# Attention and two feed-forward layers in one kernel: column halves from even and odd tiles, value sums on 32 array columns, denominators by tensor_reduce

## The chip, the cores and the metric

One Trainium2 chip, one NeuronCore of it. The metric is the device time of one execution of the whole program in microseconds (us). The kernel before takes 609.03 us, the median of 3 runs (608.67 to 610.44).

## The reference

Everything is float32. Three stages follow one another; `B, H, S, D = 2, 8, 768, 64`, so there are 1536 tokens of 512 values.

```python
k_sum = k.reshape(B, H, nb, 32, D).max(axis=3)          # nb = 24 blocks of 32 keys
v_sum = v.reshape(B, H, nb, 32, D).mean(axis=3)
scores = concat(where(abs(i - j) < 16, scale * q @ k.T, -1e9), scale * q @ k_sum.T + log(32))
a = exp(scores - max); a = a / (sum(a) + 1e-9)
x = a @ concat(v, v_sum)                                # attention, [1536, 512]
y = silu(x @ w_gate) * (x @ w_val) @ w_out              # hidden width 1536
h = y @ w_in                                            # hidden width 2048
out = where(h >= 1, h, where(h <= -1, 0, (h + 1)**2 / 4)) @ w_out2
```

## The kernel before

**Attention.** A group is one batch, 768 tokens, in 12 tiles of 64 queries (`QT`). A tile sees 96 keys and 24 block sums, padded to 128 columns. For tile `s` (0 to 11 in group 0) the engines do in turn: `first_scores` on TensorE (L536), `mask_scores` on VectorE (L1117), four `exponentials` on ScalarE with their totals (L843), `inverses` on VectorE (L1125, which adds 1e-9 to the totals by a tensor_scalar, and L1127), `normalise` on GpSimd (L1394), `transposes` on TensorE (L557), `copy_trans` on ScalarE (L856) and `values` on TensorE (L579). `values` wants in rows 96 to 127 of its operand `v_s` (group 0) or `v_a` (group 1) the 24 block means of v. `value_sums` (L517) makes these: six matmuls of 128 by 512 per group, with a selection matrix `sel` as weights, into rows 96 to 127 of one PSUM bank. For group 0 they stand in the PE's order at tiles 3, 4 and 5 (`SUMS_WITH`), and VectorE copies them out (`place_v_sum`, L1105 and L1106); three DMAs of the SP queue (L387) spread them to the other tiles. For group 1 they stand between the first products of the feed-forward stage, and ScalarE copies them (L826) and issues two DMAs for them (L831).

**Feed-forward.** Each group's x, 512 by 768, is cut into 2 by 2 blocks, rows by rows and columns by columns (`T` is 384 tokens), and multiplied by a 7-product scheme with sums and differences of blocks. `raw` holds x. `x_sum` (L1155, VectorE) makes the differences T1 to T4, `x_part_hi` (L884, ScalarE) rounds each of seven blocks to float32r in `x_hi`, and `x_part_lo` (L1163, VectorE) leaves the remainder in `x_lo`; each product is six matmuls (L589). The products of a unit `u` are p1, p2, p4 of the unit before, p6, p3 of the unit before, p5 and p7, in the order of the loop. The first one of a phase waits for the block of x that it reads (`x_needed`). In group 0 the columns 0 to 383 are tiles 0 to 5, so that B11 and B21 (all that p1 and p2 read) are ready after tile 5.

There are four phases `k`: group 0 and group 1 through the gated layer, then both through the second. While phase 0 runs, the attention of group 1 (tiles 12 to 23) runs between its products. Each phase ends in the second matmul of its layer (L698 for k below 2, L726 after), and `evacuate` copies the accumulators out of PSUM. In phases 2 and 3 these are six tiles of 128 tokens by 512, in `y_out`.

**The SP queue.** All loads and stores but the two of L831 are issued by SP, in one written order. `load_w(u)` (L429) brings the weights of a unit in two transfers, into one of three buffers; `load_wout` (L437) the second matmul's; `store(k)` (L444) issues six stores of 128 rows of 2 KB from `y_out` as the accumulators come out. `store(2)` stands in SP's order before the loads of units 3 to 7 of phase 3, `store(3)` at the end.

```python
def store(k):
    g = k % 2
    for j in range(len(ACC2)):
        sp.wait_ge(*evacuated(k, j))
        row = g * S + j * P
        sp.dma_start(out[row:row + P, :], y_out[g][:, j]).then_inc(stored, 16)
```

**ScalarE and VectorE in a unit.** ScalarE does for unit `u` in turn: `u3_copy(u-1)`, `p1_copy(u)`, `w_hi_a(u+1)` (which waits for `load_w(u+1)`), `take_c21(u-1)`, `u2_copy(u)`. p7(u) waits for `u2_copy(u)`.

Of the kernel before, what the change touches and what calls it, by code (L numbers as in the profile page):

```python
# [9 lines left out]
ACT = mybir.ActivationFunctionType  # L10
# [3 lines left out]
P = 128  # L14
# [21 lines left out]
SEL0 = WIN + (VCH - 1) * (P // BLOCK)  # L36
# [13 lines left out]

T = S // 2
T_A = T - 2 * QT
# [18 lines left out]
SLOTS_T = 9  # L71
# [38 lines left out]
def build(nc, q_t, k_t, v_rows, w1, w2, out):  # L110
    ctx = ExitStack()
    with ctx:
# [22 lines left out]
        prob_tx = at("prob_tx", 18432, [SLOTS_T - 5, PAIRS, P])  # L135
# [3 lines left out]
        k_raw_b = [at(f"k_raw_b{c}", o, [S // SUB // 3 * PAIRS * SUB]) for c, o in enumerate((152576, 156672, 189440))]  # L139
# [14 lines left out]
        v_sum = at("v_sum", 193536, [B, DM])  # L154
        masked = at("masked", 197632, [2, PAIRS, COLS])
        sel = at("sel", 201728, [SEL0 - WIN + P])
# [6 lines left out]
        total = at("total", 212544, [RING, PAIRS])  # L163
        denom = at("denom", 212608, [RING, PAIRS])
        inv = at("inv", 212672, [RING, PAIRS])
        half = at("half", 212736, [1])
# [86 lines left out]
        v_pair_sums = sem("v_pair_sums")  # L253
        v_first_sums = [sem(f"v_first_sums{j}") for j in range(len(SUMS_AT))]
        v_late_loaded = [sem(f"v_late_loaded{j}") for j in range(2)]
        v_late_sums = [sem(f"v_late_sums{j}") for j in range(2)]
# [87 lines left out]
        def x_count(k, m, part=1):  # L344
            if k == 0:
                return {X_B11: 1, X_B21: 2, X_T2: 3 + part, X_T1: 5 + part}.get(m, m + 3)
            return 7 * k + m + 3

        def t_count(k, i, part=1):
            return 4 * k + i + 3 if k or i >= 2 else i + 1 + 2 * part  # L350

        def part_cols(k, m, part):
            return slice(0, T) if k or m not in (X_T1, X_T2) else (slice(0, T_A), slice(T_A, T))[part]

# [7 lines left out]
        def _(sp):  # L362
# [10 lines left out]
            def load_v_tok(b):  # L373
                src = v_rows[b, WINDOW:WINDOW + S, :].rearrange("(c p) d -> p c d", p=P)
                for c in range(0, VCH, 2):
                    sp.dma_start((v_tok_a, v_tok_b)[b][:, c:c + 2], src[:, c:c + 2]).then_inc(v_tok_loaded[b][c // 2], 16)
# [5 lines left out]

            def place_first_sums(j):
                if j == 0:
                    sp.wait_ge(v_sum_ready, 1)
                c0, c1 = SUMS_AT[j]
                sp.dma_start(v_s[WIN:, c0:c1], v_sum[WIN:, 0].unsqueeze(1).to_broadcast([P - WIN, c1 - c0, DM])  # L387
                             ).then_inc(v_first_sums[j], 16)
# [63 lines left out]
            load_q(2)  # L452
            load_q(3)
            load_v(0)
            load_q(4)
            load_v(1)
            load_q(5)
            load_v(2)
            load_w(1)
            load_v(3)  # L460
            place_first_sums(0)
            place_first_sums(1)
            place_first_sums(2)
# [14 lines left out]
            load_late(7)  # L478
            load_w(4)
# [28 lines left out]
        def _(pe):  # L508
            def value_sums(b, i):
# [9 lines left out]
                if i == VCH - 1:  # L519
# [40 lines left out]
            def values(s, dst):  # L560
                v, c0 = v_slots(s // 2)
                r = c0 + s % 2
                if s % 2 == 0:
                    pr = s // 2
                    pe.wait_ge(v_first_loaded[pr] if pr < FIRST else v_late_loaded[pr % 2], v_count(pr))
                    if s == 0:
                        pe.wait_ge(v_pair_sums, 1)
                    for j, (c0, _) in enumerate(SUMS_AT):
                        if s == c0:
# [923 lines left out]
```

## Time and profile before

| | us |
|---|---|
| median of 3 runs | 609.03 |
| lowest and highest run | 608.67, 610.44 |
| the profiled execution, its own time | 608.4 |
| its span | 606.3 |
| TensorE matmul busy | 586.3 |
| VectorE busy | 469.5 |
| ScalarE busy | 363.2 |
| GpSimd busy | 86.4 |

The span runs from the first to the last recorded event; 2.1 us of the execution's own time lie around it. The granted TensorE clock has a mean of 0.997. Busy times are shares of the span by engine; weight loads of TensorE (PEld) overlap its matmuls.

### The profile page before, as it was taken

To read this page: it belongs to the slowest core of one execution; us is meant where nothing else is said; L and a number is where in the kernel's file an instruction comes from. 1 tells how busy PE (TensorE), PEld (TensorE's weight loads), DVE (VectorE), ACT (ScalarE), POOL (GpSimd) and SP (SyncE) were. 2 spreads that over 40 slices of the span, in tenths; PEclk is the share of its full clock that TensorE was granted. 3 is DMA by queue.
4 is the path that set the end of the run, shared out by engine and by line. 5 is a ranking of instruction groups with operands and counts; after the bars stand their busy time and mean duration, and the time that the engine had idled before them with its cause. 6 is when DMAs were issued, how large, how long until landed. Compare 5 with 4: busy or idle time off the path is not lost.

```text
span 606.3 us, 10568 instructions
## 1 busy us (share of the span) xinstructions
PE 586.3 (97%) x3912; PEld 540.4 (89%) x3912; DVE 469.5 (77%) x906; ACT 363.2 (60%) x733; POOL 86.4 (14%) x80
## 2 busy tenths in 40 slices
PE   3989999999999999999999999999999999999997
PEld 3667789989899999999999999998878899998886
DVE  6789788988585667778776767998998479979833
ACT  4776888888755456666634545664655456655522
POOL 3760232432300002232210000000000000000000
PEclk9989999999999999999999999999999999999999
DMA  9985442442122112223212111321111323002212
GB/s 331 242 302 159 129 138 79 132 131 97 53 61 62 53 35 70 71 69 122 88 53 70 53 36 69 122 88 46 60 52 53 139 70 122 2 35 73 67 53 104
DMA packets 31330, 57.50 MB, mean 95 GB/s; under 512 B 3184, under 2 KB 5744, under 8 KB 31280
## 3 DMA queue, kind: packets, MB, share of 16 engines
q1 hardware_dynamic: 31120, 56.57, 28.8%
q8 instruction: 31, 0.51, 0.4%
q10 hardware_dynamic: 160, 0.26, 0.2%
q14 instruction: 19, 0.16, 0.1%
HBM read 52.23 MB, written 3.15 MB: 91 GB/s over the span
## 4 chain that ended last, share of the span: by engine, by line
PE 82%; DVE 9%; ACT 5%; issue 2%; DMA 1%; POOL 0%; ACTq 0%; POOLq 0%; SPq 0%; DVEq 0%
PE ps L589 45%; PE ps L726 18%; PE ps L698 15%; ACT prob_s L843 1%; DVE hid_lo L1231 1%; PE ps L557 1%; PE ps L579 1%; DMA k_raw<-k_t_dram 1%; PE ps L550 1%; DVE rel L1237 1%; PE ps L517 1%; DVE h L1240 1%; DVE x_lo L1163 1%; DVE wout_lo L1225 1%; ACT prob L843 1%
## 5 line engine op out<-in xcount | busy, mean ns | idle before, releaser
L589 PE MATMUL ps<-x_hi,w_hi 128*128 128x384 f32 x560 | 192.1, 343 | 1.3 <-DVE h L1219 0.4
L589 PE MATMUL ps<-x_lo,w_hi 128*128 128x384 f32 x560 | 187.4, 335 | 0.0
L589 PE MATMUL ps<-x_hi,w_lo 128*128 128x384 f32 x560 | 187.2, 334 | 0.0
L589 PEld LDWEIGHTS ps<-x_hi,w_hi 128*128 128x128 f32 x560 | 105.1, 188 | 6.0 <-issue 3.7
L589 PEld LDWEIGHTS ps<-x_hi,w_lo 128*128 128x128 f32 x560 | 105.2, 188 | 1.1 <-issue 1.0
L589 PEld LDWEIGHTS ps<-x_lo,w_hi 128*128 128x128 f32 x560 | 105.1, 188 | 0.0
L962 ACT ACTIVATE wout_hi<-wout_raw 128x512 fp32r<-128x512 f32 x56 | 35.3, 631 | 95.1 <-PE ps L726 52.0
L726 PE MATMUL ps<-wout_hi,hid_hi 128*128 128x512 f32 x192 | 74.8, 390 | 0.8 <-DVE wout_lo L1225 0.8
L726 PE MATMUL ps<-wout_hi,hid_lo 128*128 128x512 f32 x192 | 75.2, 392 | 0.1
L726 PE MATMUL ps<-wout_lo,hid_hi 128*128 128x512 f32 x192 | 74.8, 389 | 0.0
L1225 DVE TENSOR_TENSOR wout_lo<-wout_raw,wout_hi 128x512 fp32r<-128x512 f32 x56 | 39.4, 704 | 40.1 <-ACT wout_hi L962 39.6
L1404 POOL TENSOR_TENSOR h<-part,silu 128x384 f32<-128x384 f32 x36 | 47.8, 1333 | 135.7 <-ACT silu L954 90.2
L698 PE MATMUL ps<-hid_lo,wout_hi 128*128 128x384 f32 x192 | 64.5, 336 | 0.6 <-DVE hid_lo L1231 0.6
L698 PE MATMUL ps<-hid_hi,wout_hi 128*128 128x384 f32 x192 | 64.3, 335 | 0.7 <-DVE wout_lo L1225 0.7
L698 PE MATMUL ps<-hid_hi,wout_lo 128*128 128x384 f32 x192 | 64.2, 334 | 0.0
L1188 DVE TENSOR_TENSOR w_lo<-w_sum,w_hi 128x1024 fp32r<-128x1024 f32 x39 | 47.5, 1219 | 14.7 <-ACT w_hi L898 14.7
L1231 DVE TENSOR_TENSOR hid_lo<-h,hid_hi 128x768 fp32r<-128x768 f32 x56 | 53.5, 956 | 1.5
L975 ACT ACTIVATE hid_hi<-h 128x768 fp32r<-128x768 f32 x56 | 46.6, 833 | 2.4 <-DVE h L1240 2.4
L898 ACT ACTIVATE w_hi<-w_sum 128x1024 fp32r<-128x1024 f32 x40 | 42.2, 1055 | 7.4 <-PE ps L589 5.1
L726 PEld LDWEIGHTS ps<-wout_hi,hid_lo 128*128 128x128 f32 x192 | 36.0, 188 | 8.6 <-DVE hid_lo L1231 1.2
L726 PEld LDWEIGHTS ps<-wout_hi,hid_hi 128*128 128x128 f32 x192 | 36.0, 188 | 8.3 <-issue 1.1
L726 PEld LDWEIGHTS ps<-wout_lo,hid_hi 128*128 128x128 f32 x192 | 36.0, 188 | 7.5
(119 smaller groups left out, 925.6 us busy)
## 6 DMA issues: line engine op xcount, KB each, us to landing
w_raw<-w_dram SPq DMA_DIRECT2D x80, 256.0 KB, 2.9
wout_raw<-w_dram SPq DMA_DIRECT2D x56, 256.0 KB, 2.6
out_dram<-y_out SPq DMA_DIRECT2D x12, 256.0 KB, 2.1
v_s<-v_rows_dram SPq DMA_DIRECT2D x6, 384.0 KB, 11.9
v_a<-v_rows_dram SPq DMA_DIRECT2D x6, 384.0 KB, 3.7
v_tok_a<-v_rows_dram SPq DMA_DIRECT2D x3, 512.0 KB, 7.9
k_raw_b<-k_t_dram SPq DMA_DIRECT2D x3, 512.0 KB, 7.5
v_tok_b<-v_rows_dram SPq DMA_DIRECT2D x3, 512.0 KB, 9.4
```

Of the source, the lines that this page charges most:

```text
L517: last = nc.tensor.matmul(v_sum_ps[b][:], sel[:, c0:c0 + P], (v_tok_a, v_tok_b)[b][:, i], start=i == 0, stop=i == VCH - 1)
L589: last = nc.tensor.matmul(dst, lhs, rhs, start=start and kk == 0 and i == 0, stop=kk == 1 and i == 2, skip_group_check=not start)
L698: last = nc.tensor.matmul(bank[ACC1[j]][:, 0:T], lhs, rhs, start=i == 0 and e == 0, stop=ends and e == 2)
L726: last = nc.tensor.matmul(bank[ACC2[j]][:], lhs, rhs, start=i == 0 and e == 0, stop=ends and e == 2)
L843: last = nc.scalar.activation(prob_of(s)[:, a], masked[:, s % 2, a], ACT.Exp, scale=-1.0, bias=neg_max[:, c, a:a + 1], accum_out=total[:, ...
L898: nc.scalar.activation(w_hi[:, u % 2, W_S2:W_S4 + 1], w_sum[:], ACT.Copy).then_inc(ws_hi, 1)
L962: nc.scalar.activation(wout_hi[:, n % 2], wout_raw[:, n % RAWS], ACT.Copy).then_inc(wout_hi_ready, 1)
L975: nc.scalar.activation(hid_hi[:, n % 2], h[:, c], ACT.Copy).then_inc(hid_hi_ready, 1)
L1188: nc.vector.tensor_tensor(w_lo[:, u % 2, W_S2:W_S4 + 1], w_sum[:], w_hi[:, u % 2, W_S2:W_S4 + 1], ALU.subtract).then_inc(ws_lo, 1)
L1225: nc.vector.tensor_tensor(wout_lo[:, n % 2], wout_raw[:, n % RAWS], wout_hi[:, n % 2], ALU.subtract).then_inc(wout_lo_ready, 1)
L1231: nc.vector.tensor_tensor(hid_lo[:, n % 2], h[:, c], hid_hi[:, n % 2], ALU.subtract).then_inc(hid_lo_ready, 1)
L1404: nc.gpsimd.tensor_tensor(dst, part[:, u % 2, c], silu[:, c], ALU.mult).then_inc(h_pool, 1)
```

## The change

1. **Order of tokens.** In a group's `raw`, columns 0 to 383 now hold the even tiles and 384 to 767 the odd ones. So `first_copy_out` and `late_copy_out` write other columns, and every block of x needs tiles from all over the group. The result comes out in that order, and `store` puts each 128 rows back in two runs of 64 rows, 128 rows apart.
2. **Token operands of phase 0** are made in two column ranges (`PARTS`, the tiles of pairs 0 to 3 and of pairs 4 and 5), each for groups of blocks at once: B11 with B21, then all four differences, then B22.
3. **Value sums** are made on 32 array columns: three steps of four matmuls of 32 by 256, each in another 32 rows of PSUM, at tiles 2 and 3 for group 0. One copy of 128 by 256 takes them out into `v_part`, and four DMAs of 12 or 20 partitions put them where they belong. For group 1 these are SP's too, behind `load_late(7)`.
4. **Denominators**: the totals stand beside a constant 1e-9, and a tensor_reduce adds the two in place of the tensor_scalar.
5. GpSimd's weight sums of unit 0 come ahead of tile 0, SP loads `v_s` in another order, and some buffers lie elsewhere (`prob_tx`, `k_raw_b`).

```diff
-T_A = T - 2 * QT
+PARTS = (slice(0, 4 * QT), slice(4 * QT, T))
+PART_PAIRS = (4, 6)
+X_GROUPS = ((0, 2), (2, 6), (6, 7))
+HI_ORDER = ((0, 0), (0, 1), (1, 0), (1, 1), (0, 2), (1, 2))
+LO_ORDER = ((0, 0), (1, 0), (0, 1), (1, 1), (0, 2), (1, 2))
-SUMS_WITH = {3: (0, 1), 4: (2, 3), 5: (4, 5)}
-SUMS_AT = ((2, 4), (4, 8), (8, TILES))
+SUMS_WITH = {2: (0, 1), 3: (2,)}
+SUMS_AT = ((0, 6), (6, TILES))
...
+            def place_sums(b, dst, ready):
+                for j in range(4):
+                    half, y = divmod(j, 2)
+                    n = P - WIN - VHALF if half else VHALF
+                    row = WIN + half * VHALF
+                    part_of = v_part[BLOCK * j:BLOCK * j + n, b].unsqueeze(1).to_broadcast([n, dst.shape[1], DM // 2])
+                    sp.dma_start(dst[row:row + n, :, y * (DM // 2):(y + 1) * (DM // 2)], part_of).then_inc(ready, 16)
...
             def store(k):
                 g = k % 2
                 for j in range(len(ACC2)):
                     sp.wait_ge(*evacuated(k, j))
-                    row = g * S + j * P
-                    sp.dma_start(out[row:row + P, :], y_out[g][:, j]).then_inc(stored, 16)
+                    half, c = divmod(j, T // P)
+                    rows = out[g * S + (4 * c + half) * QT:g * S + (4 * c + half + 1) * QT, :]
+                    both = bass.AP(rows.tensor, rows.offset, [(2 * QT * DM, 2), (DM, QT), (1, DM)])
+                    sp.dma_start(both, y_out[g][:, j]).then_inc(stored, 16)
...
-                if i % 2 == 0:
-                    pe.wait_ge(v_tok_loaded[b][i // 2], 16)
-                c0 = SEL0 - WIN - i * (P // BLOCK)
-                last = nc.tensor.matmul(v_sum_ps[b][:], sel[:, c0:c0 + P], (v_tok_a, v_tok_b)[b][:, i],
-                                        start=i == 0, stop=i == VCH - 1)
+                pe.wait_ge(v_tok_loaded[b][i], 16)
+                c0 = SEL0 - i * (P // BLOCK)
+                for j in range(4):
+                    half, y = divmod(j, 2)
+                    last = nc.tensor.matmul(v_sum_ps[b][BLOCK * j:BLOCK * j + BLOCK, 0:DM // 2], sel[:, c0:c0 + BLOCK],
+                                            (v_tok_a, v_tok_b)[b][:, half * (VCH // 2) + i, y * (DM // 2):(y + 1) * (DM // 2)],
+                                            start=i == 0, stop=i == VCH // 2 - 1)
...
-                c = (s - LAST_A) * QT
+                c = s % 2 * T + (s - LAST_A) // 2 * QT
                 nc.scalar.activation(raw[1][:, :, c:c + QT], tile_out(AT1), ACT.Copy).then_inc(late_out, 1)
...
-                nc.vector.tensor_scalar(denom[:, c], total[:, c], 1e-9, None, ALU.add).then_inc(denom_ready, 1)
+                nc.vector.tensor_reduce(denom[:, c], total[:, c], AX.X, ALU.add).then_inc(denom_ready, 1)
...
+            def x_first_lo(part, group):
+                dve.wait_ge(x_hi_ready, HI_ORDER.index((part, group)) + 1)
+                if group:
+                    dve.wait_ge(scores_done, LAST_A)
+                lo, hi = X_GROUPS[group]
+                nc.vector.tensor_tensor(x_lo[:, lo:hi, :, PARTS[part]], x_first(raw[0], part, group),
+                                        x_hi[:, lo:hi, :, PARTS[part]], ALU.subtract).then_inc(x_lo_ready, 1)
```

**Three places in the order.** First SP, from the second matmul's loads of phase 2 to the end. Before:

```order
L437 DMA wout_raw<-w_dram 128x512 x13
L444 DMA out_dram<-y_out_55 128x512 x6
L429 DMA w_raw<-w_dram 128x512 x10
L437 DMA wout_raw<-w_dram 128x512 x16
L444 DMA out_dram<-y_out_56 128x512 x6
```

And changed:

```order
L465 DMA wout_raw<-w_dram 128x512 x13
L474 DMA out_dram<-y_out_55 2x64x512 x6
L457 DMA w_raw<-w_dram 128x512 x10
L465 DMA wout_raw<-w_dram 128x512 x16
L474 DMA out_dram<-y_out_56 2x64x512 x6
```

Nothing has moved; the destination of each store has three dimensions, 2 by 64 by 512, where it had 128 by 512. Its source is still 128 partitions by 512.

Second, VectorE where group 0's attention ends and its x operands are made (`k_sum` rows are the key maxima of group 1). Before:

```order
L1101 TENSOR_REDUCE k_sum<-k_raw_b_70 128x4x8
L1125 TENSOR_SCALAR denom<-total 128x4
L1127 RECIPROCAL inv<-denom 128x4
...
L1163 TENSOR_TENSOR x_lo<-raw_53,x_hi 128x768
...
L1163 TENSOR_TENSOR x_lo<-raw_53,x_hi 128x768
L1101 TENSOR_REDUCE k_sum<-k_raw_b_71 128x4x8
L1155 TENSOR_TENSOR t_first<-raw_53 128x2x256
```

And changed:

```order
L1165 TENSOR_TENSOR t_first<-raw_53 128x2x256
L1165 TENSOR_TENSOR t_first<-raw_53,t_first 128x2x256
L1173 TENSOR_TENSOR x_lo<-raw_53,x_hi 128x4x256
L1121 TENSOR_REDUCE k_sum<-k_raw_b_71 128x4x8
...
L1165 TENSOR_TENSOR t_first<-raw_53 128x2x128
L1165 TENSOR_TENSOR t_first<-raw_53,t_first 128x2x128
L1173 TENSOR_TENSOR x_lo<-raw_53,x_hi 128x4x128
...
L1173 TENSOR_TENSOR x_lo<-t_first,x_hi 128x8x256
```

The remainder that the first product needs stood right behind the copy of pair 3; it is now complete only with the range of 128 columns, behind the four differences of the first range, a key maximum and the copy of pair 5.

Third, TensorE at tiles 3 and 4 of group 0 (`q_b` are queries, `ident` rows transposes). Before:

```order
L536 MATMUL ps<-k_raw,q_a 64x96 x4
L536 MATMUL ps<-k_sum,q_a 64x32 x4
L557 MATMUL ps<-ident,prob_s 128x128 x4
L517 MATMUL ps<-v_tok_a,sel 128x512 x2
L536 MATMUL ps<-k_raw,q_b 64x96 x4
```

And changed:

```order
L569 MATMUL ps<-k_raw,q_a 64x96 x4
L569 MATMUL ps<-k_sum,q_a 64x32 x4
L549 MATMUL ps<-v_tok_a,sel 32x256 x4
L590 MATMUL ps<-ident,prob_s 128x128 x4
L569 MATMUL ps<-k_raw,q_b 64x96 x4
```

The value sums stand ahead of the first transposes instead of behind three of them.

## Rows read from the trace of the kernel before

**Rows 1.** Busy time by stretch (us): engine busy, PEclk, DMA share, GB/s.

```profile
18.00:21.00 3.00, 3.00 (x41) 1.72 (x41) 1.47 (x11) 2.13 (x9) 2.47 (x4) 1.00 1.06 308
...
24.00:27.00 3.00, 3.00 (x93) 2.61 (x96) 2.65 (x19) 2.01 (x8) 1.12 (x3) 1.00 0.68 141
27.00:30.00 3.00, 3.00 (x94) 2.62 (x88) 2.67 (x14) 3.00 (x12) 1.95 (x3) 1.00 0.98 253
...
40.00:41.00 1.00, 1.00 (x17) 0.88 (x14) 1.00 (x2) 1.00 (x2) 0.57 (x1) 0.50 1.05 385
...
43.00:44.00 1.00, 1.00 (x16) 0.69 (x13) 1.00 (x2) 0.00 (x0) 0.00 (x0) 1.00 0.14 51
```

**Rows 2.** Timeline of PE, 0 to 75 us: start, duration, what.

```profile
14.82 1.88 PE L517 MATMUL ps<-v_tok_a,sel 128*128 128x512 f32 x4
...
24.69 0.69 PE L579 MATMUL ps<-prob_ts,v_s 128*64 128x64 f32 x16
...
43.33 1.98 PE L517 MATMUL ps<-v_tok_b,sel 128*128 128x512 f32 x4
...
48.56 0.74 PE L589 MATMUL ps<-x_hi,w_hi 128*128 128x384 f32 x1
...
56.01 0.67 PE L550 MATMUL ps<-k_a,q_a 64*64 64x128 f32 x16
...
62.77 0.63 PE L557 MATMUL ps<-ident,prob 128*128 128x128 f32 x4 [0.99 <-POOL prob L1394]
```

**Rows 3.** Timeline of ACT: the copy behind the last exponentials of group 0.

```profile
38.37 0.58 ACT L856 ACTIVATE prob_ts<-ps 128x512 f32<-128x512 f32 x1
```

**Rows 4.** Timeline of DVE: a denominator that waits, and work behind it.

```profile
32.25 0.88 DVE L1125 TENSOR_SCALAR denom<-total 128x4 f32<-128x4 f32 x1 [1.17 <-ACT prob_s L843]
...
41.91 0.94 DVE L1163 TENSOR_TENSOR x_lo<-raw,x_hi 128x768 fp32r<-128x768 f32 x1
...
46.62 0.42 DVE L1155 TENSOR_TENSOR t_first<-raw 128x256 f32<-128x256 f32 x1
...
49.39 1.21 DVE L1101 TENSOR_REDUCE k_sum<-k_raw_b 128x32 f32<-128x1024 f32 x1
...
55.30 0.95 DVE L1163 TENSOR_TENSOR x_lo<-raw,x_hi 128x768 fp32r<-128x768 f32 x1
```

**Rows 5.** Timeline of POOL at the same time.

```profile
30.75 2.37 POOL L1436 TENSOR_TENSOR w_lo<-w_sum,w_hi 128x1024 fp32r<-128x1024 f32 x1
```

**Rows 6.** DMA issues, 0 to 110 us: KB each, median us to landing.

```profile
k_a<-k_sum SPq DMA_DIRECT2D x2, 128.0 KB, 4.6
```

**Rows 7.** Timeline of SP: the stores and the weights behind them.

```profile
476.72 3.83 SPq L444 DMA_DIRECT2D out_dram<-y_out  x6
480.59 28.61 SPq L429 DMA_DIRECT2D w_raw<-w_dram  x10
```

**Rows 8.** The last six stores: timeline of SP.

```profile
600.37 3.83 SPq L444 DMA_DIRECT2D out_dram<-y_out  x6
```

**Rows 9.** DMA, 600.7 to 605.8 us: 40 slices, packets, queue and issues.

```profile
DMA  0000899995789999999999998999899999999300
...
DMA packets 864, 1.57 MB, mean 308 GB/s; under 512 B 96, under 2 KB 96, under 8 KB 864
...
q1 hardware_dynamic: 864, 1.57, 82.5%
...
out_dram<-y_out SPq DMA_DIRECT2D x6, 256.0 KB, 2.1
```

**Rows 10.** The whole span: the queue of ScalarE's two DMAs.

```profile
q10 hardware_dynamic: 160, 0.26, 0.2%
```

**Rows 11.** Timeline of ACT in unit 2 of phase 3.

```profile
493.43 0.63 ACT L891 ACTIVATE w_hi<-w_raw 128x512 fp32r<-128x512 f32 x1
```

**Rows 12.** Timeline of PE in the same unit: the first matmul of p7.

```profile
498.04 0.33 PE L589 MATMUL ps<-x_hi,w_hi 128*128 128x384 f32 x1
```

More of the change, by code:

```diff
@@ L162, in build @@
         neg_max = at("neg_max", 212480, [RING, PAIRS])
[L163 to L166, printed above, removed]
+        total = at("total", 212544, [RING, PAIRS, 2])
+        denom = at("denom", 212672, [RING, PAIRS])
+        inv = at("inv", 212736, [RING, PAIRS])
+        half = at("half", 212800, [1])
         ps = ctx.enter_context(nc.psum_tensor("ps", [P, 8, 512], F32))
@@ L341, in evacuated, with x_count, t_at, x_first @@
             return (evac_act, evac_dve)[j % 2], (0, 4, 8, 11)[k] + j // 2 + 1
-        def x_count(k, m, part=1):
+        def x_count(k, m):
             if k == 0:
-                return {X_B11: 1, X_B21: 2, X_T2: 3 + part, X_T1: 5 + part}.get(m, m + 3)
-            return 7 * k + m + 3
+                group = [lo <= m < hi for lo, hi in X_GROUPS].index(True)
+                return 1 + max(LO_ORDER.index((part, group)) for part in range(2))
+            return 7 * k + m
         def t_count(k, i, part=1):
-            return 4 * k + i + 3 if k or i >= 2 else i + 1 + 2 * part
-        def part_cols(k, m, part):
-            return slice(0, T) if k or m not in (X_T1, X_T2) else (slice(0, T_A), slice(T_A, T))[part]
+            return 4 * k + i + 5 if k else 4 * part + i + 1
+        def t_at(i):
+            return (1, 0, 2, 3)[i]
+        def x_first(raw0, part, group):
+            cols = PARTS[part]
+            if group == 0:
+                return raw0[:, :, cols].rearrange("p (m k) c -> p m k c", m=2)
+            if group == 1:
+                return t_first[:, :, :, cols]
+            return raw0[:, 2:4, T + cols.start:T + cols.stop].unsqueeze(1)
         def block_of(k, i):
@@ L748, in _ @@
                 first_scores(s)
+                for i in SUMS_WITH.get(s, ()):
+                    value_sums(0, i)
                 now = VALUES_AT.get(s, ())
@@ L755, in _ @@
                     first_values(i)
-                for i in SUMS_WITH.get(s, ()):
-                    value_sums(0, i)
             first_transposes(LAST_A - 3)
@@ L859, in late_copy_out, with x_first_hi, x_part_hi @@
                 act.wait_ge(attn_done, s + 1)
-                c = (s - LAST_A) * QT
+                c = s % 2 * T + (s - LAST_A) // 2 * QT
                 nc.scalar.activation(raw[1][:, :, c:c + QT], tile_out(AT1), ACT.Copy).then_inc(late_out, 1)
-            def x_part_hi(k, m, part=1):
+            def x_first_hi(part, group):
+                act.wait_ge(first_out, PART_PAIRS[part])
+                if group == 1:
+                    act.wait_ge(t_ready, t_count(0, 3, part))
+                lo, hi = X_GROUPS[group]
+                nc.scalar.activation(x_hi[:, lo:hi, :, PARTS[part]], x_first(raw[0], part, group), ACT.Copy).then_inc(x_hi_ready, 1)
+            def x_part_hi(k, m):
                 r = raw[k % 2]
                 if m in (X_B11, X_B21, X_B22):
-                    if k == 0:
-                        act.wait_ge(first_out, FIRST if m == X_B22 else FIRST // 2)
-                    elif k == 1:
+                    if k == 1:
                         act.wait_ge(late_out, LAST_A)
@@ L1439, in _ @@
             pool.wait_ge(selected, steps)
+            for step in range(3):
+                first_weight_sums(0, step)
             for s in range(LAST_A):
                 normalise(s)
-                if 1 <= s <= 3:
-                    first_weight_sums(0, s - 1)
-                elif s == 4:
+                if s == 1:
                     first_w_lo_a()
-                elif s == 5:
+                elif s == 3:
                     first_w_lo_b()
```

202 lines of the change are left out of this document (96 added, 106 removed).

## The prediction

> **What bounds the kernel now.** I read the busy time by stretch first, then the timelines of PE, ACT and DVE up to 75 us, then the SP queue and its DMAs at the two places where results are stored. Three stretches differ.
>
> *Attention of group 0, up to 39 us.* ScalarE should set the pace, and from 27 us on it does: 3.00 busy of 3.00. Before that PE holds it up: in the three stretches of 3 us from 18 to 27 (the first and the last are shown) ScalarE is busy 2.13, 2.13 and 2.01 [rows 1]. What PE does there is value sums, 1.88 us for two matmuls of 128 by 512 [rows 2].
>
> *The passage to the feed-forward stage, 39 to 76 us.* VectorE works without a gap on x operands; the matmuls follow it. PE runs on a granted clock of 0.50 for some 3 us here, which is its level of 1.2 GHz, after two thin microseconds, and is back at 1.00 by 43 us [rows 1].
>
> *From 76 us to the end* PE is the bound, and little waits. So this part has a fixed length, unless a change starves it. The stores hide under it in phase 2; in phase 3 they are the tail: SP issues the last six from 600.37 us on [rows 8], and the data move from 601.2 to 605.4 (the slices from the fifth to the 38th) [rows 9].
>
> **The change part by part.**
>
> *Value sums.* Two of the old matmuls cost 1.88 us [rows 2], so one of the new, with half the columns, 0.47 us, and a group has twelve. If the four of a step run side by side, a group costs 3 x 0.47 = 1.4 us in place of 5.6; if not, the same 5.6. That matmuls on different array columns do overlap shows in the value matmuls: 8 with 64 columns would be 8 x 64/512 x 0.94 = 0.94 us one behind the other, and take 0.69 [rows 2]. I take 1.4.
>
> *Attention of group 0.* ScalarE's waits of 18 to 27 us go (0.87 + 0.87 + 0.99 = 2.7 us). So do the long denominators: the one at 32.25 lasts 0.88 us and ends at 33.13, when the GpSimd instruction of 30.75 ends (33.12) [rows 4, 5]. A tensor_reduce of 128 by 8 has no row here; between nothing gained and all of that wait, 0 to 0.7 us for each such case, I take 0.5 once. ScalarE then is done with the exponentials of tile 11 at about 35 instead of 38.4 [rows 3].
>
> *The passage.* Here 3.4 us are mostly given back. p1 of unit 0 needed the first half of the tokens, and now needs all. Behind the copy of pair 3, at 35.4, VectorE has to do: three copies (0.6 each), four differences of 512 columns (0.6), the remainder of 1024 (1.1), a key maximum (1.1), two differences of 256 (0.35) and a remainder of 512 (0.6), 7.7 us, and 0.5 of waiting for GpSimd. The prices go by columns: 768 cost 0.95, 256 cost 0.42, a key maximum 1.21 [rows 4], less some 0.08 by which neighbours overlap. p1 starts at 43.8. p6 needs another 4.7 us of VectorE's work and starts at 48.5, where it started at 48.56 before [rows 2]. So nearly nothing is won up to there. The two value sums behind it shrink by 0.4 us each. The scores of tile 12 (56.01 before [rows 2]) now wait for the last key maximum, done at about 51.0, and its transfer, 4.6 us [rows 6]: 55.6, a gain of 0.4. VectorE has then finished the x operands (before at 56.2, the end of the remainder at 55.30 [rows 4]), so tile 12's softmax runs without delay, and its transpose moves from 62.77 [rows 2] to 60.5. Its values wait for four small DMAs of SP. I keep **2.0 us** of gain. Ends: VectorE's finish moves by 5.2 us (56.2 to 51.0), a gain of at most 5; and a loss of 1.5, if PE, idle from 39.3 to 43.8, starts the stage at 1.2 GHz and the loss does not fit into its 2 us of slack ahead of p6.
>
> *The stores.* This is the term that decides. Today six stores are 864 packets, 144 each: 128 rows and 16 more. ScalarE's two transfers are 160, 80 each: 64 rows and 16 more [rows 9, 10]. So each is cut into sixteen, over all 16 DMA engines. In each transfer of before that I looked at the outermost count is the same on both sides (128, 96 or 32 partitions). The new store has 128 outermost at its source and 2 at its destination. No row shows such a transfer. Bounds: sixteen engines as today, or two. I take **two**, as that is the only outermost count by which both sides can be cut. The six stores take 0.825 x 16 x 5.1 us = 67.3 engine-us for 1.57 MB [rows 9], so one engine moves 23.4 GB/s, and two move the six stores in 67.3 / 2 = **33.7 us**, in place of 4.2.
>
> The Trainium skill, page "DMA: Bandwidth & Descriptors", section "Why a DMA increments its semaphore by 16 and not by 1", says that a transfer is split by the largest number up to 16 that divides the slowest dimension of both sides, so two here. With the page's 27 GiB/s of an engine the stores would take 27 us, by my estimate, and the total would be 642 us. The packets of both transfers agree with the split; none shows a small one.
>
> *At the end*: the data end at 601.2 + 33.7 = 634.9 instead of 605.4: **+29.5 us**.
>
> *In the middle*: `store(2)` is issued from 476.72, the data start 0.85 us later (as at the end), at 477.6, and end at 511.3. Behind it SP issues the weights of unit 3 of phase 3, from 480.59 [rows 7]. They use all engines, the two busy ones among them, and queue there behind the stores; then 2 x 16 KB for each engine at 23.4 GB/s, 1.4 us, and 0.6 to land: 513.3. ScalarE wants them at 493.43 [rows 11] and stands; behind `w_hi_a` stand `take_c21` and `u2_copy` (1.4 us for the three), and p7 of unit 2 waits for the last. PE gets there at 498.04 [rows 12] and goes on at 514.7: 16.7 us. Its clock will be at 1.2 GHz then, as it was around 40 us; there it lasted some 3.4 us (it is at 1.00 again in the stretch from 43 [rows 1]), half of which is lost: 1.7. Together **+18.4 us**.
>
> *Sum*: 608.4 - 2.0 + 29.5 + 18.4 = 654.3 for the profiled execution. The median stands 0.6 above it: **655**.
>
> *Costed at nothing*: the sums of unit 0 on GpSimd (it has nothing else to do before the first denominators), the column order in the late copies (the same elements), SP's new order of loads (the value sums that it waits for are ready sooner, so the loads behind them are issued sooner too). If that cover goes, each is worth under 1 us.
>
> **The rivals.**
>
> 1. *Only the end pays.* Later loads pass the stores on the two engines, or come in time. Against it: one queue carries both. Time: 609.0 - 2.0 + 29.5 = 636.5.
> 2. *The stores still go to 16 engines*, the 128 partitions of the source setting the split. This ends on the other side, and the point is the number n of engines: the end costs 67.3/n - 4.2, the middle nothing from n = 4 on. From 11 engines up the end costs under 2 us and the gain of 2.0 wins. With 16: 607.0.
> 3. *Sixteen engines, and the clock takes the gain.* With value sums gone PE is busy for some 1.2 us of each 2.0 in tiles 4 to 7, and idle for 4.5 us ahead of p1. The granted clock fell after a stretch like that once [rows 1]. Then transposes and scores take twice as long, about ScalarE's own pace, and p1 and p2 2 us more: 610.5.
>
> The Trainium skill, page "TensorE: Matmul & The Clock Gate", Part 1, has the clock fall to half after a spell without work, which would favour 3 over 2; the row at 40 us agrees with it, and it leaves my sum as it is, where the loss stands already.
>
> **How the numbers follow.** Forecast 0.80; rival 1 0.07; rival 2 0.09; rival 3 0.04. A measurement of this kernel tells 0.3% (1.8 us) from nothing: faster 0.08 (most of rival 2), same 0.03, slower 0.89. The range of the forecast itself goes by the speed of one engine. Both places take the six stores' time: at 27 us for them (one engine a quarter faster) the total is 642, and at 39 us (a seventh slower) 666; 2 us more for the front's ends. With rival 1 it reaches down to 636. Left out are rivals 2 and 3, 0.13, and the tails. Range **636 to 668**.
>
> **What would show it.** Two engines: the landing time of `out_dram` rises from 2.1 us to over 20 for the last; the six stores have 130 packets each; the DMA share after 605 us is near 2/16; a wait of PE of some 16 us on the weights of unit 3 of phase 3, with a granted clock of 0.5 behind it. The front: value sums of about 0.5 us a step; p1 of unit 0 near 43.8, and PE's steady stretch starting 2 us earlier. I would be wrong if stores keep 144 packets; partly, if the weights of unit 3 land on time.

## Result and the profile after

| | before | changed |
|---|---|---|
| median | 609.54 us (4 runs, 608.67 to 610.44) | 659.05 us (4 runs, 657.2 to 663.36) |
| profiled execution: own time, span | 608.4, 606.3 us | 660.64, 658.9 us |
| granted clock, mean | 0.997 | 0.953 |

Ratio **1.0814** (95% interval 1.0787 to 1.084): 49.5 us slower. The forecast was 655.0 (636 to 668), slower.

Three marks divide both spans: the first issue of `store(2)`, that of `store(3)`, and the end. The timeline of SP of the changed kernel has them; [rows 7, 8] are the same rows of before.

```profile
16.50 3.49 SPq L405 DMA_DIRECT2D v_s<-v_part  x4
...
21.82 3.27 SPq L405 DMA_DIRECT2D v_s<-v_part  x4
...
484.21 20.12 SPq L474 DMA_DIRECT2D out_dram<-y_out  x6
504.37 29.38 SPq L457 DMA_DIRECT2D w_raw<-w_dram  x10
...
624.93 19.96 SPq L474 DMA_DIRECT2D out_dram<-y_out  x6
```

| part | before | changed | difference | predicted |
|---|---|---|---|---|
| front, to `store(2)` | 476.72 | 484.21 | +7.5 | -2.0 |
| middle, to `store(3)` | 123.65 | 140.72 | +17.1 | +18.4 |
| end | 5.93 | 33.97 | +28.0 | +29.5 |

The end, in the DMA view of 624 to 658.9 us: 40 slices of busy tenths, then their rates, packets, queue and issues. It answers to [rows 9].

```profile
DMA  0010111111111111111111111111111111111110
GB/s 0 0 19 28 28 38 52 52 52 49 49 52 52 61 52 52 52 52 52 47 52 52 52 52 52 52 52 52 49 49 52 52 52 52 52 52 52 52 49 2
DMA packets 781, 1.58 MB, mean 45 GB/s; under 512 B 12, under 2 KB 12, under 8 KB 780
...
q1 hardware_dynamic: 780, 1.57, 12.0%
```

The data move from the third slice to the 39th, 625.7 to 658.0: 32.3 us, where 4.2 were. The same 1.57 MB now go at 52 GB/s in the full slices; over its whole window, idle slices included, this view has a mean of 45 where [rows 9] have 308. The small packets are 12 for six stores, two a store, where [rows 9] have 96, sixteen a store. The engines were busy for 0.120 x 16 x 34.9 = 67.0 engine-us, as before (67.3): the work is the same, done by two instead of sixteen.

The middle, in the timelines of ACT and PE. They answer to [rows 11, 12].

```profile
519.18 0.63 ACT L917 ACTIVATE w_hi<-w_raw 128x512 fp32r<-128x512 f32 x1 [18.16 <-DMA w_raw<-w_dram]
```

```profile
520.62 0.69 PE L620 MATMUL ps<-x_hi,w_hi 128*128 128x384 f32 x1 [14.93 <-ACT part L954]
521.11 0.52 PE L620 MATMUL ps<-x_hi,w_lo 128*128 128x384 f32 x1
```

ScalarE waits 18.2 us for the weights behind the stores, PE 14.9 us for ScalarE, and its matmuls then take 0.52 us instead of 0.33: the granted clock is 0.50 from 520 to 524 us, and 1.00 again from 526 on. Against the first issue of `store(2)`, p7 starts 15.1 us later than before (36.4 us behind it, not 21.3); the other 2.0 us of the middle come with this clock.

The front, by stretch (busy time of PE, PEld, DVE, ACT, POOL, then granted clock, DMA share, GB/s). It answers to [rows 1].

```profile
21.00:24.00 3.00, 2.47 (x68) 2.16 (x68) 1.18 (x10) 1.92 (x9) 0.69 (x2) 0.83 1.06 153
24.00:27.00 3.00, 1.67 (x19) 1.58 (x20) 1.27 (x10) 1.02 (x6) 1.71 (x2) 0.50 1.01 218
27.00:30.00 3.00, 3.00 (x59) 2.49 (x59) 0.85 (x2) 2.46 (x10) 0.00 (x0) 0.54 1.07 162
```

And what PE did there, and at p1 of unit 0 (the first row answers to the first of [rows 2]):

```profile
12.27 1.26 PE L549 MATMUL ps<-v_tok_a,sel 128*32 128x256 f32 x16
14.15 0.64 PE L549 MATMUL ps<-v_tok_a,sel 128*32 128x256 f32 x8
...
21.51 0.40 PE L569 MATMUL ps<-k_raw,q_b 64*64 64x96 f32 x8 [2.01 <-DMA q_b<-q_t_dram]
25.34 1.12 PE L610 MATMUL ps<-prob_ts,v_s 128*64 128x64 f32 x16 [1.36 <-issue]
...
34.05 0.38 PE L569 MATMUL ps<-k_raw,q_d 64*64 64x96 f32 x3
36.62 0.43 PE L569 MATMUL ps<-k_raw,q_d 64*64 64x96 f32 x3 [2.20 <-issue]
...
52.74 0.66 PE L620 MATMUL ps<-x_hi,w_hi 128*128 128x384 f32 x1 [4.57 <-issue]
53.19 0.52 PE L620 MATMUL ps<-x_hi,w_lo 128*128 128x384 f32 x1
```

DVE at tile 11's denominator, first before and then changed, with the copy of pair 3 behind it:

```profile
38.50 0.74 DVE L1125 TENSOR_SCALAR denom<-total 128x4 f32<-128x4 f32 x1 [0.31 <-ACT prob_s L843]
...
43.56 0.16 DVE L1143 TENSOR_REDUCE denom<-total 128x4 f32<-128x8 f32 x1 [0.93 <-ACT prob_s L865]
...
43.85 0.66 DVE L1150 COPY raw<-ps 128x512 f32<-128x512 f32 x1
```

The value sums did become cheap, 1.9 us in place of 5.6. But ScalarE, which should have gained by it, is busy 1.92 and 1.02 of 3.00; PE waits for transfers, its clock goes to 0.50, and the DMA engines are busy all the time while they move 153 to 218 GB/s, where the first of [rows 1] has 308 at the same share. The denominator of tile 11 comes at 43.56 us, not at 38.50, and tile 12's transposes at 70.11, not at 62.77. So 5.1 us of the front are lost in group 0's attention and 2.3 in the passage.

The wait before 25.34 ends when the value sums are there. The DMA view in steps of 1 us counts rows of 1 KB, which in this stretch are those of the sums alone: of the 384 rows for tiles 0 to 5, issued from 16.50 on, the first moves after 18 us, 383 have moved by 24 and the last by 25.

The wait of 2.20 us at 36.62 is of another kind: it stands inside the scores of one tile, where the program has no wait. It comes up again below.

### The profile page after: what moved, and what is told of

It reads as the page before. It is cut to its first block, busy times and chain, and to the rows that moved or that the text cites. A ratio compares the mean times of both kernels' runs of the same rounds, so it can differ in the third digit from the quotient of the medians.

```text
span 658.9 us, 10625 instructions
## 1 busy us (share of the span) xinstructions
PE 587.1 (89%) x3936; PEld 543.1 (82%) x3936; DVE 465.8 (71%) x905; ACT 363.0 (55%) x730; POOL 86.6 (13%) x80
## 4 chain that ended last, share of the span: by engine, by line
PE 78%; DVE 5%; SPq 4%; DMA 4%; issue 3%; ACT 1%; POOL 0%; POOLq 0%; ACTq 0%; DVEq 0%
PE ps L620 42%; PE ps L757 16%; PE ps L729 14%; SPq L474 3%; DMA q_b<-q_t_dram 2%; PE ps L610 2%; PE ps L590 2%; DMA w_raw<-w_dram 1%; DVE hid_lo L1264 1%; PE ps L583 1%; PE ps L569 1%; SPq L457 1%; DVE rel L1270 1%; DVE h L1273 1%; DVE t_late L1190 1%
## 5 line engine op out<-in xcount | busy, mean ns | idle before, releaser
L620 PE MATMUL ps<-x_hi,w_hi 128*128 128x384 f32 x560 | 192.6, 344 | 19.9 <-ACT part L954 14.9
L988 ACT ACTIVATE wout_hi<-wout_raw 128x512 fp32r<-128x512 f32 x56 | 35.3, 631 | 95.1 <-PE ps L757 52.0
```

Source lines behind the costliest of these rows:

```text
L620: last = nc.tensor.matmul(dst, lhs, rhs, start=start and kk == 0 and i == 0, stop=kk == 1 and i == 2, skip_group_check=not start)
L988: nc.scalar.activation(wout_hi[:, n % 2], wout_raw[:, n % RAWS], ACT.Copy).then_inc(wout_hi_ready, 1)
```

## The experiments

Of the forecast, the two store terms had to be shown and the front explained. Times are medians; "front" is the first issue of `store(2)` in the profiled execution, against 476.72. The front of one and the same program moves by up to 2.5 us from one execution to another (the changed kernel, split stores and split middle are the same there: 484.21, 484.92 and 486.67), so medians weigh more than a single front.

### Split stores

```diff
-                    both = bass.AP(rows.tensor, rows.offset, [(2 * QT * DM, 2), (DM, QT), (1, DM)])
-                    sp.dma_start(both, y_out[g][:, j]).then_inc(stored, 16)
+                    for i in range(2):
+                        r0 = g * S + (4 * c + half + 2 * i) * QT
+                        sp.dma_start(out[r0:r0 + QT, :], y_out[g][i * QT:(i + 1) * QT, j]).then_inc(stored, 16)
```

> The changed kernel with each of its twelve stores made as two transfers of 64 partitions, each to one run of 64 rows of the output, instead of one transfer of 128 partitions whose destination has three dimensions. Output is the same. Theory (the three-dimensional destination spreads a store over two DMA engines only): the end falls back from 34.0 us behind the first issue of the second group of stores to about 6, the stretch between the two groups of stores from 140.7 to about 123.6, and what is left is the later start of the first group (+7.5): 659.0 - 28.0 - 17.1 = 614 us (611 to 618). Rival (the stores are slow for another reason, the 512-column rows or the W loads beside them): the time stays within 3 us of 659.

Measured: **619.91 us** (617.46 to 621.88; before beside it 608.91; ratio 1.0166, 1.0128 to 1.0205).

```profile
484.92 7.62 SPq L474 DMA_DIRECT2D out_dram<-y_out  x12
...
608.58 7.52 SPq L474 DMA_DIRECT2D out_dram<-y_out  x12
```

The middle is 608.58 - 484.92 = 123.66, as before: the whole term is gone. The end is 618.2 - 608.58 = 9.6, so 24.4 of 28.0 are gone; 3.7 stay, since the twelve issues in a row take 7.52 us where the six of before took 3.83. That, and a front 0.7 us later, are 4.4 of the 6 us between 620 and the expected 614; the other 1.6 are that 614 was reckoned from the median, 659.05, with terms from an execution of 660.64.

### The new destination alone, in the kernel before

```diff
-                    row = g * S + j * P
-                    sp.dma_start(out[row:row + P, :], y_out[g][:, j]).then_inc(stored, 16)
+                    half, c = divmod(j, T // P)
+                    rows = out[g * S + (4 * c + half) * QT:g * S + (4 * c + half + 1) * QT, :]
+                    both = bass.AP(rows.tensor, rows.offset, [(2 * QT * DM, 2), (DM, QT), (1, DM)])
+                    sp.dma_start(both, y_out[g][:, j]).then_inc(stored, 16)
```

> The kernel before with nothing changed but the destination of its stores, which takes the changed kernel's three-dimensional form (so output rows come out in another order than the reference's). Theory (two engines): end +28 and middle +17, no change at the front: 609.5 + 45 = 654.5 us (651 to 658). Rival (the stores cost this only together with the later or denser work of the changed kernel): under 640.

Measured: **654.38 us** (653.71 to 655.21; ratio 1.0734, 1.0698 to 1.077).

```profile
477.98 18.24 SPq L446 DMA_DIRECT2D out_dram<-y_out  x6
...
618.56 18.20 SPq L446 DMA_DIRECT2D out_dram<-y_out  x6
```

Front +1.3, middle 140.58 (+16.9), end 652.5 - 618.56 = 33.9 (+28.0). The destination alone carries 45 of the change's 50 us.

### Only the first group split

```diff
+                    if k == 2:
+                        for i in range(2):
...
+                        continue
```

> The changed kernel with only the first group of six stores split into 64-partition transfers, the last group left as it is. Theory: the middle term goes, the end term stays: 659.0 - 17.1 = 642 us (639 to 645), with no wait for w_raw at the start of the last phase and the granted clock of the 12 us behind it at 1.0. Rival (the last group of loads and stores takes up what is gained): above 650.

Measured: **643.25 us** (642.04 to 646.19). The middle is 610.32 - 486.67 = 123.65, the end 644.4 - 610.32 = 34.1. The two terms are independent: the second group takes its full 34 us though the first was quick. The granted clock is 1.00 from 486 to 506 us, so the low clock of the middle goes with the wait.

### The value sums of before, in the changed kernel

Split stores, and beside the lines below `load_v_tok`, `copy_v_sum`, the late sums and the order of loads as in the kernel before. A group has six products; the expectation says eight by mistake.

```diff
-SUMS_WITH = {2: (0, 1), 3: (2,)}
-SUMS_AT = ((0, 6), (6, TILES))
+SUMS_WITH = {3: (0, 1), 4: (2, 3), 5: (4, 5)}
+SUMS_AT = ((2, 4), (4, 8), (8, TILES))
...
+                last = nc.tensor.matmul(v_sum_ps[b][:], sel[:, c0:c0 + P], (v_tok_a, v_tok_b)[b][:, i],
+                                        start=i == 0, stop=i == VCH - 1)
...
+                nc.vector.tensor_copy(v_s[WIN:, 0:2], v_sum_ps[0][WIN:, :].unsqueeze(1).to_broadcast([P - WIN, 2, DM])
```

> The changed kernel with split stores and with the value sums of the kernel before: eight 128-column products of all 512 value columns, placed by its larger transfers and by a copy on DVE, loads in its order; the token ranges and the denominators stay as changed. Theory A (the placing transfers, 1 KB rows on few DMA engines and ahead of the loads, make the front late): the front comes back to that of the kernel before or better, 607 us (604 to 610). Rival B (the token ranges, the longer operand work or the denominators cost the front its time): as the split stores alone, about 614.

Measured: **616.78 us** (614.82 to 618.81; ratio 1.0117, 1.0076 to 1.0158, which overlaps that of the split stores). Neither theory: 3.1 us go, not 13 nor 0. The timeline of PE in this kernel, of p1 and p6 of unit 0 and the transposes of tile 12:

```profile
47.71 0.41 PE L608 MATMUL ps<-x_hi,w_hi 128*128 128x384 f32 x1 [2.68 <-issue]
...
52.39 0.44 PE L608 MATMUL ps<-x_hi,w_hi 128*128 128x384 f32 x1 [0.64 <-DVE x_lo L1174]
...
65.15 0.63 PE L576 MATMUL ps<-ident,prob 128*128 128x128 f32 x4 [0.43 <-POOL prob L1428]
```

Tile 11's denominator starts at 38.50 us, exactly as in before. From there p1 takes until 47.71 instead of 44.75, and tile 12's transposes come at 65.15 instead of 62.77; the front is +2.8. So the token ranges cost 2 to 3 us of their own, in the passage, where the forecast had them (by this profiled execution, 614.82 us, the fastest of the four; GpSimd's earlier weight sums of unit 0 are in it too and were not run alone), and 3.9 are the stores' issues. The split version lies 11.0 us above before; going back to the old sums takes off 3.1 of them in the medians, and 5.4 of the front in the profiled executions (484.92 to 479.51).

### Order of loads, and placing in two steps

In the changed kernel with split stores:

```diff
             load_q(2)
+            load_q(3)
             load_v(0)
-            load_v(1)
-            load_q(3)
+            load_q(4)
+            load_v(1)
+            load_q(5)
             load_v(2)
             place_first_sums(0)
-            load_q(4)
             load_v(3)
-            load_q(5)
             place_first_sums(1)
```

> The changed kernel with split stores, and with the query loads and the first three value loads all issued ahead of the wait for v_part and the placing transfers, as in the kernel before. Split stores alone gave 619.9 us, with the old value sums too 616.8. Theory O (the front is late because q_d and the fourth value load stand behind the wait for v_part on SP, so the DMA engines idle before it and are crowded after it): 615 us (613 to 617), waits for q_b and q_d gone. Rival P (the placing transfers themselves, 768 rows of 1 KB on at most 12 engines, take the time wherever they stand): 618 to 621, and DMA rates below 200 GB/s while they run.

Measured: **619.79 us** (619.4 to 622.29), against 619.91 with split stores alone. Theory O falls: the wait for `q_b` is gone, and the one at the first values grows.

```profile
26.82 1.12 PE L610 MATMUL ps<-prob_ts,v_s 128*64 128x64 f32 x16 [5.01 <-issue]
```

The rows of 1 KB show it: the 384 for the first six tiles are issued from 16.63 us on, hardly later than in the changed kernel, but with more loads ahead of them, and move between 20 and 26 us, not between 18 and 25. What is left of the earlier waits, 0.77 us at 18.52, stands inside a tile's scores again.

On top of it, the placing in two steps:

```diff
-                    sp.dma_start(dst[row:row + n, :, y * (DM // 2):(y + 1) * (DM // 2)], part_of).then_inc(ready, 16)
+                    sp.dma_start(v_sum[row:row + n, y * (DM // 2):(y + 1) * (DM // 2)], part_of).then_inc(v_sum_placed, 16)
...
+                    sp.wait_ge(v_sum_placed, 64)
...
+                sp.dma_start(v_s[WIN:, c0:c1], v_sum[WIN:].unsqueeze(1).to_broadcast([P - WIN, c1 - c0, DM])
```

> The same as the order experiment, but the sums are placed in two steps: four small transfers gather them once into one 32-partition row block of 2 KB rows (64 rows of 1 KB), and from there whole 2 KB rows are copied to the twelve tiles, as the kernel before does. Output is the same. Rival P (the 768 rows of 1 KB on few engines cost the time): 2 to 4 us below the order experiment. Theory O: within 1.5 us of the order experiment, since the rows are not what is waited for; the added step of about 2 us before the first value products may show.

Measured: **622.23 us** (621.39 to 624.18): slower by 2.4, so rival P, as I had put it, falls too. The timeline of SP shows the price of the second step: the whole rows can only be sent at 23.47, 3.6 us behind the last small issue.

```profile
16.70 3.22 SPq L407 DMA_DIRECT2D v_sum<-v_part  x4
23.47 0.73 SPq L415 DMA_DIRECT2D v_s<-v_sum  x1
```

### The new value sums alone, in the kernel before

The reverse: `value_sums`, `v_part`, `place_sums` and `place_late_sums` on SP of the change; stores, token order and denominators old.

```diff
-SUMS_WITH = {3: (0, 1), 4: (2, 3), 5: (4, 5)}
-SUMS_AT = ((2, 4), (4, 8), (8, TILES))
+SUMS_WITH = {2: (0, 1), 3: (2,)}
+SUMS_AT = ((0, 6), (6, TILES))
...
-                nc.vector.tensor_copy(v_s[WIN:, 0:2], v_sum_ps[0][WIN:, :].unsqueeze(1).to_broadcast([P - WIN, 2, DM])
...
+                    sp.dma_start(dst[row:row + n, :, y * (DM // 2):(y + 1) * (DM // 2)], part_of).then_inc(ready, 16)
```

> The kernel before with the value sums of the change alone (three steps of four products on 32 columns, 1 KB rows placed by SP in both groups) and the loads ahead of the wait for v_part; its stores, token order, operands and denominators are the old ones. Theory O (the sums are cheaper on TensorE, and with the queue's order kept they cost nothing elsewhere): 607 us (605 to 609). Rival P (the placing transfers cost more than the 4.2 us of TensorE they save): 610 to 614.

Measured: **613.76 us** (613.46 to 614.29; ratio 1.0067, 1.0044 to 1.0089): they cost 4.5 us where I had given them a gain. And with the two-step lines of the run before on top:

> The kernel before with the change's value sums, placed in two steps as in the two-step experiment. Theory O: within 1 us of the one-step version. Rival P: below it by 2 us or more, 606 to 609, and then faster than both kernels.

Measured: **618.0 us** (616.82 to 619.1), worse again. The first of the two, at the values of tile 0:

```profile
26.68 1.12 PE L591 MATMUL ps<-prob_ts,v_s 128*64 128x64 f32 x16 [4.79 <-issue]
```

In before that matmul runs at 24.69 without a wait [rows 2]. There DVE copies the sums into `v_s` for the first two tiles itself (L1106). In the change every row of sums comes by DMA, from 16.50 us on. This made theory S.

### Without the first six tiles' sums

Against the new value sums alone, with the one placing behind the fourth load of v:

```diff
-SUMS_AT = ((0, 6), (6, TILES))
+SUMS_AT = ((6, TILES),)
...
+            nc.gpsimd.memset(v_s[WIN:, 0:6], 0.0).then_inc(zeroed, 1)
```

> The kernel before with the change's value sums, but the sums of the first six tiles left out: GpSimd fills their rows with zeros at the start, and only the transfers for tiles 6 to 11 are made. With all transfers it was 613.8 us, with values(0) behind 4.8 us of idle TensorE and 6 us at a granted clock of 0.50. Theory S: that wait and the low clock go, and the time falls to 606 to 610. Rival P (the 1 KB rows load the DMA engines, and all behind them is late): half of the rows stay, so 611 to 613, with q_d still waited for.

Measured: **610.6 us** (609.27 to 612.46; ratio 1.0022, 1.0008 to 1.0035). PE's timeline and the busy time by stretch of this kernel:

```profile
22.73 0.69 PE L591 MATMUL ps<-prob_ts,v_s 128*64 128x64 f32 x16
...
30.99 0.38 PE L550 MATMUL ps<-k_raw,q_d 64*64 64x96 f32 x3
34.27 0.30 PE L550 MATMUL ps<-k_raw,q_d 64*64 64x96 f32 x3 [2.91 <-issue]
```

```profile
24.00:27.00 3.00, 2.00 (x60) 1.72 (x60) 1.98 (x14) 3.00 (x16) 2.72 (x3) 1.00 1.08 168
```

Theory S said 606 to 610, rival P 611 to 613; it lies between them, nearer to S. The values of tile 0 are at 22.73 without a wait, the clock stays at 1.00 until 35 us and ScalarE is busy 3.00 of 3.00. That takes back about 3 of the 4.5 us (1.6 are left against before, 609.04 beside it). It takes half of the transfers away too, and a load of v goes ahead of the others, so it does not separate the wait from their load on the DMA engines. And though PE has 3.7 us less to do, nothing is won on before: tile 11's denominator is at 40.87 us instead of 38.50, behind a wait of 2.91 us and a clock of 0.50 from 36 to 39.

That wait is inside the scores of one tile, behind the third of eight matmul records of a group that the program lets run without a wait, and all the queries for it landed by 22 us (issued at 8.71, at most 12.9 us to landing). The DMA view of this stretch has a queue of another kind, `q8 instruction`, which moves a packet of 16 KB now and then. Here such a packet starts at 31.9, takes 1.1 us, and PE goes on 1.3 us later. The same holds for the waits of this kind in the other kernels (start of the packet, its time, PE's next matmul): changed kernel 34.0, 1.3, 36.62; split stores 33.0, 1.3, 35.91; order of loads 35.3, 1.3, 38.03; new sums in before 34.5, 1.5, 37.50. In before the packet starts at 29.2, and no wait is seen. This points to the program's own instructions, which come late behind the data; no run tests it.

### Sums on four column sets, copied by DVE

```diff
+                    for j in range(4):
+                        last = nc.tensor.matmul(v_sum_ps[0][BLOCK * j:BLOCK * j + BLOCK, 0:P], sel[:, c0:c0 + BLOCK],
+                                                v_tok_a[:, i, j * P:(j + 1) * P], start=i == 0, stop=i == VCH - 1)
```

> The kernel before with its first value sums alone made in another way: four products of 32 array columns beside each other, each for 128 of the 512 value columns, and all six token chunks added in place, so that each set of 32 partitions holds all 24 sums of its columns. DVE copies these to the last 32 partitions of v_sum and of the first two tiles of v_s, in four pieces each, and the other tiles get 2 KB rows by DMA as before. The sums stand at tiles 2 and 3 as in the change. Output is the same. Theory S (the change's sums cost their time by reaching v_s through a DMA only, which values(0) waits for): no wait at values(0), and the 4 us of TensorE saved show in part: 607 us (605 to 609). Rival T (moving the sums earlier or the narrow products cost the time, whatever places them): 611 to 614.

Measured: **615.45 us** (613.6 to 617.19; ratio 1.0097, 1.0078 to 1.0116). Theory S gave 607, so it is not enough. DVE's timeline, then PE's:

```profile
16.80 1.20 DVE L1114 COPY v_sum<-ps 32x128 f32<-32x128 f32 x4
18.02 1.73 DVE L1117 COPY v_s<-ps 32x256 f32<-32x256 f32 x4
```

```profile
24.93 1.12 PE L587 MATMUL ps<-prob_ts,v_s 128*64 128x64 f32 x16
...
31.08 0.68 PE L587 MATMUL ps<-prob_ts,v_s 128*64 128x64 f32 x15
34.80 0.27 PE L587 MATMUL ps<-prob_ts,v_s 128*64 128x64 f32 x1 [3.05 <-issue]
```

The wait at tile 0 is gone as expected, but eight small copies hold DVE for 2.9 us between two tiles' scores (ScalarE is busy 0.58 of 3.00 from 18 to 21 us), the clock is 0.55 from 24 to 27, and a later group of values waits 3.05 us ahead of the last of its 16 matmul records. That is again a wait inside a group: a packet of `q8 instruction` starts at 32.3 and takes 1.1 us, and PE goes on at 34.80. Rival T's range, 611 to 614, is missed too.

### Denominators alone, in the kernel before

```diff
-                nc.vector.tensor_scalar(denom[:, c], total[:, c], 1e-9, None, ALU.add).then_inc(denom_ready, 1)
+                nc.vector.tensor_reduce(denom[:, c], total[:, c], AX.X, ALU.add).then_inc(denom_ready, 1)
```

> The kernel before with the denominators alone made as in the change, by one TENSOR_REDUCE over sums and a constant column in place of TENSOR_SCALAR. Theory: the 0.74 to 0.88 us instructions fall to 0.16, but what follows them is mostly hidden: 609 (608 to 610). Rival (DVE is on the path in the attention of batch 0, where TENSOR_SCALAR waits for GpSimd's port): 606 to 607.5.

Measured: **608.74 us** (12 runs; before beside it 609.04; ratio 0.9989, 0.9975 to 1.0002): no change, the span is 606.3 in both. In the changed kernel the instruction lasts 0.16 us where [rows 4] has 0.88, and nobody waited for the difference.

### Last half stores on two queues

```diff
+ACT_STORES = ((0, 1), (2, 1), (4, 0), (4, 1), (5, 1))
...
+                                if jj == j or (jj == 5 and j == 4):
+                                    act.wait_ge(*evacuated(k, jj))
+                                    store_half(act, k % 2, jj, i)
```

> The changed kernel with split stores and the old value sums, and five of the last twelve half stores issued by ACT's queue behind its own copies, seven by SP. Output is the same. Theory (with split stores the end is set by twelve issues of 0.64 us in a row on SP): the last issue starts 4.5 us behind the first instead of 7.1, the end falls from 9.8 us behind the first issue to about 7, and the time from 616.8 to 614 us (612.5 to 615.5). Rival (the end is set by how fast the DMA engines write 64-row transfers): the end stays at 9.8 us and the time at 616 to 618.

Measured: **614.49 us** (613.22 to 615.94; ratio 1.0074, 1.0048 to 1.01; the one-queue version had 1.0117, 1.0076 to 1.0158). SP's and ACT's timelines of the end:

```profile
603.48 5.15 SPq L350 DMA_DIRECT2D out_dram<-y_out  x7
```

```profile
606.20 1.92 ACTq L350 DMA_DIRECT2D out_dram<-y_out  x3
```

The end is 612.2 - 603.48 = 8.7 us instead of 9.8. The last issue is over 5.2 us behind the first instead of 7.7, 2.5 us earlier, but only 1.1 of it reaches the end: both theories hold in part. The median's 2.3 is mostly within what the intervals leave open.

## Why the prediction was right, and where it was not

**The stores: right, mechanism and size.** "Bounds: sixteen engines as today, or two", and it took two: two small packets a store, 780 packets as forecast, 52 GB/s. The end was put at +29.5 and was +28.0, the middle at +18.4 and was +17.1; the new destination alone gives 45.5 us in the medians, and splitting takes the middle back whole. Both terms were 1.3 to 1.5 us too large for one reason, the six stores' time: put at 33.7 us, measured 32.3. The rule of the Trainium skill, page "DMA: Bandwidth & Descriptors", section "Why a DMA increments its semaphore by 16 and not by 1", that had spoken for two engines agrees with these rows. By the page's 27 GiB/s (29 GB/s) the stores would have been quicker than they were: the full slices show 26 GB/s an engine, so the trace's own row gave the better size. Rival 1 fell with the wait of 18.2 us for `w_raw`, rivals 2 and 3 with the 52 GB/s.

**The passage: right.** "p1 starts at 43.8", 8.4 us behind the copy of pair 3 at 35.4 (its terms add up to 8.2). With the old sums that copy is at 38.80 and p1 at 47.71, 8.9 us; in the changed kernel itself it is at 43.85 and p1 at 52.74, again 8.9. "Another 4.7 us" to p6: 4.7 with the old sums (52.39). Tile 12's transposes were put 25.1 us behind the copy (60.5) and come 26.3 behind it. The end of its range with p1 at the low clock came true in the changed kernel (0.52 us a matmul at 53.19). Only it all stood on a start that never came earlier, so what the forecast called given back was a cost of 2 to 3 us.

**The front's start: wrong in sign.** The step was "ScalarE's waits of 18 to 27 us go", 2.7 us, with ScalarE "done with the exponentials of tile 11 at about 35 instead of 38.4". The products became cheap as said (1.9 us; I had 1.4). What the step left out is how the sums reach `v_s`. I followed PE's 5.6 us and overlooked that the change also takes away DVE's direct copy for the first two tiles. Now the first rows are issued at 16.50, and the values of tile 0 wait for them: 1.36 us in the changed kernel, where 2.01 us had gone on `q_b` before, and about 5 us where `q_b` was in time. PE's clock then goes to 0.50 for some 6 us. The value sums alone cost 4.5 us in the kernel before, about 3 of it bound to the first six tiles' transfers. For the denominators the lower end of the forecast, nothing, was right, and not the 0.5 us taken.

That a cheaper PE might give nothing back even without that wait (610.6 us) could be suspected: [rows 1] have the DMA engines at 1.06, 0.68 and 0.98 of their time from 18 us to 30, and I read PE's 3.00 alone.

**The load order, costed at nothing: right** (619.79 against 619.91), though it is the waits that change place, not that they were covered.

The sum: sums 4.5 (alone, in before), ranges 2 to 3, denominators 0 make the front's 7.5, within the 2.5 us by which fronts of one program differ. The front was off by 9.5 us and the two store terms by 2.8 the other way, which together are the 6.3 by which the profiled execution (660.64) lies above its sum (654.3), within 0.4. The median lies 4 us above the forecast. For the front the forecast had allowed 2 us at its ends; that the whole stayed inside the range is owed to the room left for the engines' speed, which was hardly needed. In that it was luck.

What stays open: how the 4.5 us divide between the wait and the load of small rows on the DMA engines, and whether the waits inside groups of matmuls are for instructions. No version tried beats the kernel before; the denominators alone equal it.

## What to carry to other kernels

Before reordering what stands in partitions, write down each store's dimensions on both sides: a destination of two pieces made six stores last 32.3 us and not 4.2, and two transfers of 64 partitions each were enough to undo it but for the issues. When a product is made cheaper, follow its result to its reader: a direct copy that becomes a DMA can cost more than the product saved. And where the DMA share is near 1 beside a busy PE, as here in most stretches up to 42 us, do not book a gain from shortening PE's work until the transfers have been counted.

## What the runs showed of the hardware that I had not expected

- A transfer's small packets count its engines for placing too. The pages of two kernels that differ in four transfers, 12, 12, 20 and 20 partitions at either end, and in one memset (first all sums by DMA, then without the first six tiles'):

```profile
DMA packets 31959, 57.64 MB, mean 94 GB/s; under 512 B 3236, under 2 KB 6820, under 8 KB 31908
```

```profile
DMA packets 31530, 57.23 MB, mean 94 GB/s; under 512 B 3192, under 2 KB 6392, under 8 KB 31480
```

  384 rows of 1 KB and 3236 - 3192 = 44 small packets, which is 12 + 12 + 10 + 10: twelve engines for 12 partitions, ten for 20. Four transfers over sixteen would have had 64. The first of these kernels also shows them singly, in group 1's four placing transfers, where little else moves: 12 small packets and 48 rows of 1 KB from 68.55 to 69.35 us (12 partitions, four tiles), 10 small packets and 80 rows from 70 to 71 (20 partitions).
- SP's issue itself became slow with few engines: the median issue of a store takes 4.26 us in the changed kernel and 0.33 in before, and the six in a row 20.12 us where they took 3.83 [rows 7], the waits for the accumulators between them included. The same bytes in twelve transfers over sixteen engines took 7.62.
- PE stood still for 0.3 to 3.05 us inside groups of matmuls without a wait in the program, in kernels whose DMA engines were full of data, and the six of them that are told above ended 1.3 to 1.6 us behind the end of a 16 KB packet of the instruction queue. In before, with the packet at 29.2 us, there is none.
- A group's twelve products of 32 columns (24 records) took 1.9 us, a step of four 0.64 us, against 1.4 and 0.47 by columns alone: side by side, but not at no cost.
